# Delta-rule attention and two expert layers on one core: the first group's 32x32 inverse from two half blocks, and key products of groups 3 to 5 in the first two groups

## What is computed

```python
for t in range(S):                      # S = 768, for each batch (4) and head (8)
    y[t] = q[t] @ state
    v_old = k_n[t] @ state              # k_n is k over its norm
    state = state + beta[t] * outer(k_n[t], v[t] - v_old)
x = y                                    # [3072, 384]
P = sinkhorn(exp(x @ w_gate))            # 8 rounds
x = sum(P[:, e] * (relu(x @ w1[e]) @ w2[e]) for e in range(8))
h = x @ w_in
out = (h * cos(h)) @ w_out
```

## Time and profile before

| | us |
|---|---|
| median of 3 runs | 2217.05 (2216.68 to 2217.41) |
| the profiled execution | 2218.46 |
| its span, first to last instruction | 2216.7 |
| TensorE busy in the span | 2155.7 (97%) |
| VectorE busy | 1029.2 (46%) |
| ScalarE busy | 699.0 (32%) |

### The profile page before, as it was taken

How to read it: one execution, slowest core, us unless ns; L and a number is a source line. 1 busy time by engine, 2 the same in 40 slices (tenths; PEclk the granted TensorE clock), 3 DMA queues, 4 the chain that set the end, 5 groups by cost and what they waited for, 6 DMA issues and landing times.

```text
span 2216.7 us, 40360 instructions
## 1 busy us (share of the span) xinstructions
PE 2155.7 (97%) x15513; PEld 1778.8 (80%) x15513; DVE 1029.2 (46%) x1744; ACT 699.0 (32%) x1178; POOL 507.9 (23%) x404
## 2 busy tenths in 40 slices
PE   6789999999999999999999999999999999999999
PEld 5667778888888888888888888888888888888887
DVE  8988726432232322323223232232322348777777
ACT  4555543111111111111111111111111137666665
POOL 1000010045232332323323233232232330000000
PEclk7799999999999999999999999999999999999999
DMA  6334432011111011111111101111111100000001
GB/s 160 96 91 106 112 113 81 29 54 43 29 30 32 29 31 45 29 32 28 33 28 28 47 28 33 28 28 33 28 33 43 29 24 15 15 15 15 0 15 71
DMA packets 83113, 97.69 MB, mean 44 GB/s; under 512 B 6848, under 2 KB 68608, under 8 KB 83008
## 3 DMA queue, kind: packets, MB, share of 16 engines
q1 hardware_dynamic: 83008, 96.18, 15.8%
HBM read 82.69 MB, written 8.75 MB: 41 GB/s over the span
## 4 chain that ended last, share of the span: by engine, by line
PE 89%; DVE 9%; issue 1%; ACT 1%; DVEq 0%; ACTq 0%
PE h L712 7%; PE h L714 7%; PE h L713 7%; PE p_h L712 7%; PE p_h L714 7%; PE p_h L713 7%; PE am_y L751 4%; PE am_y L750 4%; PE am_y L752 4%; PE cy_y_y L750 4%; PE cy_y_y L751 4%; PE cy_y_y L752 4%; DVE t_leaf L1375 2%; DVE prod L1373 2%; PE o_y L750 2%; PE state_y L750 2%
## 5 line engine op out<-in xcount | busy, mean ns | idle before, releaser
L1278 POOL TENSOR_TENSOR acc<-acc,py 128x512 f32 (+1 forms) x252 | 324.3, 1318 | 745.8 <-DVE py L1585 745.8
L1143 ACT ACTIVATE hhi<-h 128x512 fp32r<-128x512 f32 x182 | 109.0, 599 | 770.8 <-PE h L714 770.8
L1548 DVE SCALAR_TENSOR_TENSOR hlo<-h,hhi 128x512 fp32r<-128x512 f32 x182 | 125.8, 691 | 474.6 <-ACT hhi L1143 474.6
L1548 DVE SCALAR_TENSOR_TENSOR hlo<-p_h,hhi 128x512 fp32r<-128x512 f32 x182 | 125.8, 691 | 403.6 <-ACT hhi L1143 403.6
L1240 POOL TENSOR_TENSOR wlo<-stage,whi (+1 forms) x114 | 147.0, 1291 | 628.8 <-ACT whi L1000 603.4
L712 PE MATMUL p_h<-xhi,whi 128*128 (+1 forms) x690 | 268.8, 390 | 0.6 <-DVE scr L1645 0.6
L712 PE MATMUL h<-xhi,whi 128*128 (+1 forms) x690 | 268.7, 389 | 0.0
L713 PE MATMUL p_h<-xlo,whi 128*128 (+1 forms) x690 | 268.5, 389 | 0.0
L714 PE MATMUL p_h<-xhi,wlo 128*128 (+1 forms) x690 | 268.4, 389 | 0.0
L713 PE MATMUL h<-xlo,whi 128*128 (+1 forms) x690 | 268.4, 389 | 0.0
L714 PE MATMUL h<-xhi,wlo 128*128 (+1 forms) x690 | 268.4, 389 | 0.0
(11 more groups left out here) (254 smaller groups left out, 3786.1 us busy)
## 6 DMA issues: line engine op xcount, KB each, us to landing
stage<-wcat SPq DMA_DIRECT2D x38, 768.0 KB, 4.4
pb<-p_scratch SPq DMA_DIRECT2D x84, 256.0 KB, 4.7
kq<-kqt SPq DMA_DIRECT2D x48, 192.0 KB, 3.5
v<-vrow SPq DMA_DIRECT2D x24, 192.0 KB, 3.9
kb<-krow SPq DMA_DIRECT2D x24, 192.0 KB, 3.6
acc<-yT SPq DMA_DIRECT2D x144, 32.0 KB, 2.1
kT<-kta SPq DMA_DIRECT2D x20, 192.0 KB, 4.5
acc<-y_scratch SPq DMA_DIRECT2D x5, 768.0 KB, 4.7
```

The source lines that it names most:

```text
L1143: act.activation(hhi[:, j, :], hps[j % 2][:, 0:TILE], ACT.Relu).then_inc(s["hhi_done"], 1)
L1278: pool.tensor_tensor(y, y, py[:, d, :], ALU.add).then_inc(s["added"], 1)
L1548: dve.scalar_tensor_tensor(out=hlo[:, j, :], in0=hps[j % 2][:, 0:TILE], scalar=0.0, in1=hhi[:, j, :].bitcast(F32), op0=ALU.max, op1=ALU.su ...
```

## The change

The first group's leaves are inverted in another way. Each 32x32 leaf is taken as two 16x16 diagonal blocks and the 16x16 block below them. VectorE inverts both diagonal blocks at once (half_blocks, a view with the two blocks as one more dimension), TensorE forms the lower block, in both layouts: joins multiplies the keys' product by the first half of z_t, ScalarE copies that into join scaled by a column of zeros and ones (lower), lower_blocks and turned_blocks multiply by z_x, and VectorE subtracts the results from z_t (lower_fixed) and z_x (turned_fixed). The three merges ahead of the first step are interleaved. GpSimd clears t_leaf and join first. The other five groups keep the 31-column elimination.

AHEAD is 3: TensorE computes key products of groups 0 to 2 in the lead. Those of 3 to 5 are placed by two tables, beside the residual of a step or after its outputs. ScalarE copies them out at the same places. In the lead, seven products of zeros (keep_up) stand where unread ones stood later; UNREAD keeps two entries, and unread waits for key copies and the first weights. The first three splits of weights and the gate's copy go from the lead to the end of step (0, 2) on ScalarE, the gate's subtraction to (1, 1) on VectorE. root(1) moves into step (0, 0), and the fourth quarter of extract(1) behind the third merged copy. The diff, cut:

```diff
-AHEAD = NG - 2
-NEAR_END = 2 + 1 + 2 * 26
-UNREAD = {(0, 0): (0, 3), (0, 1): (5, 0), (0, 2): (5, 0), (0, 3): (4, 0),
-          (1, 0): (4, 0), (1, 1): (5, 0), (1, 2): (5, 0)}
+HL = L // 2
+AHEAD = NG // 2
+KEYS_BESIDE = {(0, 1): (3, 1), (0, 2): (4, 1), (1, 0): (5, 0), (1, 1): (5, 1)}
+KEYS_AFTER = {(0, 0): (3, 0), (0, 1): (4, 0)}
+UNREAD = {(0, 3): 4, (1, 2): 5}
...
@@ sync
         for part in range(2):
-            load_kT(3, part)
+            load_kT(AHEAD, part)
         load_kq(2)
+        load_rows(2)
         load_w(0, 1, wraw)
-        load_rows(2)
         load_rows(3)
-        for part in range(2):
-            load_kT(AHEAD, part)
...
-                if g == 0 and c < 2:
-                    load_kT(NG - 1, c)
...
                 if c % 2 == 1:
                     move_y(i // 2)
+                if g == 0 and c < 2:
+                    for part in range(2):
+                        load_kT(AHEAD + 1 + c, part)
@@ tensor
+        def joins(bank, first, last):
+            for n in range(first, last):
+                for q in range(4):
+                    r, f = slice(L * q, L * q + L), L * (q % 2)
+                    mm = pe.matmul(bank[r, n * HL:(n + 1) * HL], keyed(0, n // RU)[r, n % RU, f:f + L], z_t[r, n, 0:HL],
+                                   start=True, stop=True)
+            mm.then_inc(a["join_made"], 1)
+
+        def lower_blocks(bank, first, last):
+            for n in range(first, last):
+                for q in (0, 2):
+                    r = slice(L * q, L * q + L)
+                    mm = pe.matmul(bank[r, n * HL:(n + 1) * HL], z_x[r, n, :], join[r, n, 0:HL], start=True, stop=True)
+            mm.then_inc(a["low_done"], 1)
+
+        def turned_blocks(bank, first, last):
+            for n in range(first, last):
+                for q in range(4):
+                    r = slice(L * q, L * q + L)
+                    mm = pe.matmul(bank[r, n * HL:(n + 1) * HL], join[r, n, :], z_x[r, n, HL:L], start=True, stop=True)
+            mm.then_inc(a["turned_done"], 1)
+
+        def first_inverses():
+            pe.wait_ge(a["zeroed"], 2)
+            pe.wait_ge(a["zt_half"], 1)
+            joins(cy_ps[:, 0, :], 0, 8)
+            joins(state_ps, 8, U)
+            pe.wait_ge(a["zx_first"], 1)
+            pe.wait_ge(a["join_evac"], 1)
+            pe.wait_ge(a["a_evac"], 4 * AHEAD)
+            lower_blocks(cy_ps[:, 1, :], 0, 8)
+            turned_blocks(o_ps, 0, 8)
+            pe.wait_ge(a["join_evac"], 2)
+            turned_blocks(am_ps[1], 8, 16)
+            pe.wait_ge(a["zt_fixed"], 1)
+            merge_units(0, 0, h_ps, 0, 8).then_inc(a["m_first"], 1)
+            lower_blocks(am_ps[0], 8, U)
+            pe.wait_ge(a["zx_fixed"], 1)
             pe.wait_ge(a["m_firsted"], 1)
-            merge_units(0, 1, h_ps, 0, 8).then_inc(a["m_first"], 1)
+            merge_units(0, 1, cy_ps[:, 0, :], 0, 8).then_inc(a["m_first"], 1)
+            turned_blocks(h_ps, 16, U)
+            pe.wait_ge(a["zt_fixed"], 2)
+            merge_units(0, 0, o_ps, 8, 16).then_inc(a["m_first"], 1)
...
         def unread(n):
+            pe.wait_ge(a["a_evac"], 4 * (NG - 1))
+            pe.wait_ge(s["whi_done"], 1)
             for _ in range(n):
                 pe.matmul(o_ps[:, :], w1(whi, 0, 0, 0), whi0[:, 0:TILE], start=True, stop=True)
+        def keep_up(n):
+            pe.wait_ge(a["zeroed"], 2)
+            zeros = X[:, 1, :, :].rearrange("p n i -> p (n i)")
+            for _ in range(n):
+                pe.matmul(cy_ps[:, 0, 0:2 * P], zeros[:, 0:P], zeros[:, P:3 * P], start=True, stop=True)
...
         query_products(0)
-        for g in range(2, AHEAD):
-            for m in range(2):
-                key_products(g, m)
-        pe.wait_ge(a["a_evac"], 4 * AHEAD)
-        pe.wait_ge(s["whi_done"], 1)
-        pe.wait_ge(a["leaf_chain"], NEAR_END)
-        unread(12)
-        first_merges()
-        unread(4)
+        pe.wait_ge(a["x_zeroed"], 1)
+        keep_up(4)
+        for m in range(2):
+            key_products(2, m)
+        keep_up(3)
+        first_inverses()
@@ scalar
         for r in range(4):
             products(1, r)
+        extract(1, 0, 3)
         for r in range(4):
             products(2, r)
-        extract(1)
-        for chunk in range(NT // 2):
-            split_hi(0, chunk, 0, 0, wraw)
-        for g in range(3, AHEAD):
-            for r in range(4):
-                products(g, r)
...
+        act.wait_ge(a["join_made"], 1)
+        joined(cy_ps[:, 0, :], 0, 8)
+        act.wait_ge(a["join_made"], 2)
+        joined(state_ps[:, :], 8, U)
         act.wait_ge(a["m_first"], 1)
...
+        act.wait_ge(a["m_first"], 3)
+        merged_units(0, 0, o_ps, 8, 16).then_inc(a["m_firsted"], 1)
+        extract(1, 3, 4)
...
+                if g == 0 and c == 2:
+                    act.wait_ge(s["gate_loaded"], 16)
+                    act.activation(wgr[:, :, 0, :], wgs[:, :, :], ACT.Copy).then_inc(s["gate_hi"], 1)
+                    for chunk in range(NT // 2):
+                        split_hi(0, chunk, 0, 0, wraw)
@@ vector
+        def half_blocks():
...
+            leaf_link(dve.tensor_tensor(t_half, a_half, turned(bpn.rearrange("p (a j) -> p a j", j=HL), HL), ALU.mult))
+            for j in range(1, HL - 1):
+                r = HL - 1 - j
+                t = t_half[:, :, j + 1:HL, 0:j]
+                x = prod[:, 0:2 * r * j].rearrange("p (a i c) -> p a i c", a=2, c=j)
+                leaf_link(dve.tensor_tensor(x, t_half[:, :, j + 1:HL, j:j + 1].broadcast_to([P, 2, r, j]),
+                                            turned(t_half[:, :, j, 0:j], r), ALU.mult))
+                leaf_link(dve.tensor_tensor(t, t, x, ALU.add))
...
+            dve.transpose(z_of[:, 0:HL, :], t_of[:, 0:HL, :]).then_inc(a["zt_half"], 1)
+            dve.transpose(z_x[:, :, :].rearrange("p n i -> p i n"), t_leaf[:, :, :]).then_inc(a["zx_first"], 1)
+            dve.transpose(z_of[:, HL:L, :], t_of[:, HL:L, :]).then_inc(a["zt_half"], 1)
...
         norms(0)
-        leaf_init(0)
-        leaf(1, 28)
-        leaf(28, L - 1)
-        leaf_end(0)
+        half_blocks()
+        lower_fixed(0, cy_ps[:, 1, :], 0, 8)
+        turned_fixed(0, o_ps[:, :], 0, 8)
         values(0)
+        lower_fixed(1, am_ps[0][:, :], 8, U)
+        turned_fixed(1, am_ps[1][:, :], 8, 16)
+        turned_fixed(2, h_ps[:, :], 16, U)
...
         leaf_start(1)
```

More of the change, by code:

```diff
@@ L158, in build @@
     r = [xlo_at]
-    t_leaf = inside(r, "t_leaf", [P, L, L])
+    t_leaf, t_half = leaf_buffer(r, "t_leaf")
     prod = inside(r, "prod", [P, 256])
@@ L173, in build @@
     assert r[0] <= xlo_at + 4 * EARLY * DC * TILE
+    lower = place("lower", [P, 2, L], F32, lgT_at)
+    join = place("join", [P, U, L], F32, xlo_at + 4 * DC * TILE + 4 * STEPS * HEADS * HD + 4 * HEADS * HB)
     mask_all = place("mask_all", [P, P], F32, xlo_at + 4 * DC * TILE + 4 * STEPS * HEADS * HD)
@@ L455, in key_products @@
                         k = kT[b * CT:b * CT + HD, (2 * m + c) * HEADS + par * HH + n, :]
-                        mm = pe.matmul(rows(key_bank(g, 2 * m + par), b ^ par)[:, j * CT:(j + 1) * CT], k, k, start=True, stop=True)
+                        mm = pe.matmul(rows(key_bank(2 * m + par), b ^ par)[:, j * CT:(j + 1) * CT], k, k, start=True, stop=True)
             mm.then_inc(a["a_done"], 2)
@@ L663, in step @@
                 merge(0, 3)
-            if AHEAD + g < NG and c < 2:
-                key_products(AHEAD + g, c)
+            if (g, c) in KEYS_AFTER:
+                key_products(*KEYS_AFTER[g, c])
             if c >= 2 and g + 1 < NG:
@@ L926, in scatter, with joined @@
                 scatter_units(g, q, part * 16, part * 16 + 16).then_inc(a["sc_done"], 1)
+        def joined(bank, first, last):
+            act.activation(join[:, first:last, 0:HL], bank.rearrange("p (n i) -> p n i", i=HL)[:, first:last, :], ACT.Copy,
+                           scale=lower[:, 1, 0:1]).then_inc(a["join_evac"], 1)
         def merged_units(g, stg, bank, first, last):
@@ L1090, in _ @@
                     scatter(0, 1)
[L1091 to L1093 removed]
+                if (g, c) in KEYS_AFTER:
+                    key_group, m = KEYS_AFTER[g, c]
+                    products(key_group, 2 * m)
+                    products(key_group, 2 * m + 1)
                 if c == 1 and g >= 1:
@@ L1228, in _ @@
                            pattern=[[-1, N_EXP]], channel_multiplier=1).then_inc(s["consts"], 1)
+        pool.memset(t_leaf[:, :, :], 0.0).then_inc(a["t_zeroed"], 1)
+        pool.memset(join[:, :, :], 0.0).then_inc(a["join_zeroed"], 1)
         pool.memset(X[:, :, :, :], 0.0).then_inc(a["x_zeroed"], 1)
@@ L1432, in _ @@
             dve.tensor_copy(mask[b * CT:(b + 1) * CT, :], mask_all[b * CT:(b + 1) * CT, b * CT:(b + 1) * CT]).then_inc(a["mask_cut"], 1)
+        dve.wait_ge(a["lower_made"], 2)
+        dve.transpose(lower[:, 1, :], lower[:, 0, :]).then_inc(a["lower_turned"], 1)
         first_extract(1)
```

127 lines of the change are left out of this document (79 added, 48 removed).

## The result

The changed kernel takes 2231.33 us (median of 4 runs, 2230.12 to 2232.15), the kernel before 2216.86 in the same series (2216.26 to 2217.41): 1.0065 times as long, 95% interval 1.0047 to 1.0082. It is slower by 14.5 us, where 2.4 us less were forecast. The profiled execution took 2232.15 us, its span 2230.4.

What follows compares the result with a forecast made beforehand. The scan of attention was taken as bound by VectorE, the rest by TensorE. A gain of 3.4 us at leaf_start(1) less 1.0 in (0,3) gave 2.4: 2217.05 to 2214.7 us, range 2209.5 to 2220.0.

Steps and rivals of the forecast that it cites:

- VectorE's list: First group's inverse on VectorE: elimination 7.8 us in place of 21.6; VectorE alone at leaf_start(1) 12.6 us early.
- half blocks don't do what they say on VectorE: Rival: each of the 28 elimination instructions pays 0.12 us more, 3.4 us, giving 2218.1 us; chance 0.06.
- the term of TensorE's stage: Joins to third merge on TensorE: records sum to 11.7 us, third merge at 38.4, gain 4.7 us before deductions.
- the deduction for its instruction stream: TensorE standing with nothing to wait for during the 736 records: 0.8 us, bounds 0 and 3.
- the bound that I named for the low clock: TensorE's small matmuls in the new stage: 26 ns a record at 1.2 GHz.
- TensorE becomes the bound and is slow: Rival: joins stage at 26 ns a record loses 2.8 us, 3 more in (0,3), 2222.9 us; chance 0.12.
- leaf_start(1) as the end of VectorE's wait: VectorE's leaf_start(1), waiting for ScalarE's extract, comes at 40.0 before deductions against 44.67; gain 3.4 us after them.
- the deductions: Taken off the stage's 4.7 us gain: 0.5 for low clock after TensorE's pause, 0.8 for its instruction stream.
- the moves: Key products, loads, splits and fill matmuls placed elsewhere: all at zero, except a 1.0 us loss in step (0,3).
- my upper bound of 3: Step (0,3), waiting for the first weight split: 3 us lost if the pauses stay and the clock falls.
- VectorE's saving should arrive at the end: Attention scan: every microsecond VectorE's list comes forward early reaches the end, unless a TensorE or ScalarE wait eats it.
- the forecast lead at R(0,1): Start of the residual in step (0,1): early by the same amount as leaf_start(1), 3.4 us.

Runs made afterwards that it cites:

- e1_root: Changed kernel with ScalarE's root(1) ahead of its wait for the second merge in step (0,0); 2228.67 us, 1.0050 of before.
- e3: Changed kernel with the first group's old 31-column inverse and root(1), extract(1) as before, all other moves kept; 2222.38 us, 1.0027 of before.
- e9: e3 with the gate's copy and first three weight splits back in the lead on ScalarE; 2219.81 us, 1.0014 of before.
- e15: e14 with the old 31-column inverse, so without the filled gap, its other places kept; 2217.11 us, 1.0002 of before.
- e14: e11 with key products spread over group 1, no last fill matmuls, both loads of keys 5 behind step (1,0); 2213.85 us, 0.9984 of before.
- e5: Changed kernel with VectorE doing group 1's work between its subtractions, later loads held back, splits in the lead, root(1) moved; 2220.52 us, 1.0011 of before.
- e8: e5 without lower_blocks, z_t taken from z_x by three VectorE transposes, 128 records fewer; 2216.57 us, 1.0000 of before.
- e10: Changed kernel with 64 more unread matmuls, 128 records, between joins and the first lower_blocks; 2234.29 us, 1.0078 of before.
- e2_loads: Changed kernel with five input loads issued only behind step (0,0); 2227.65 us, 1.0048 of before.
- e6: e5 without the filling, masked(0) ahead of lower_fixed(1), root(1) ahead of the second merge's wait; 2222.20 us, 1.0025 of before.
- e11: e8 with extract(2) moved behind updates(0, 2) on ScalarE; 2216.35 us, 0.9996 of before.
- e13: e11 with key products spread, no last fill matmuls, the load for (5,1) ahead of step (1,1)'s moves of y; 2219.37 us, 1.0006 of before.

## Why the prediction was wrong

**Right: VectorE's list.** The elimination was put at 7.8 us and took 7.8 (16.70 to 24.50), z_t's first half was to be ready at 26.5 and the joins to begin at 26.7 (26.6 and 26.73); subtractions of 128 and 256 elements were put at 0.3 and 0.45 and took 0.29 and 0.42. The rival "half blocks don't do what they say on VectorE" is out.

**Wrong: the term of TensorE's stage, and in it the deduction for its instruction stream.** The third merge was to end at 38.4; it ended at 50.2, 11.8 us later. Of that, 10.0 us are the four pauses, against a deduction of 0.8 with a bound of 3. The other 1.8 are the pace between them: 13.5 us for 736 records, 18.4 ns each, against 15.9. The four-quadrant records did what I took (91 in 1.41 us, 15.5 ns, even at a clock of 0.50); the two-quadrant ones, 83 in 2.19 us from 43.04, took 26 ns, the bound that I named for the low clock. I had the right row in hand, with pauses of 1.84 and 0.94 us, and took from it a sum for the whole stage, where it should have been read as a rate: between the ends of the two pauses, 89.87 and 93.84, before has 128 records as well. The windows of after between the ends of pauses show the rate (from:to, length, PE busy (count), PEclk, DMA share, GB/s):

```profile
26.70:34.67 7.97, 2.38 (x163) 0.50 0.96 270
34.67:38.56 3.89, 2.33 (x128) 0.50 0.03 11
38.56:42.02 3.46, 1.90 (x128) 0.50 0.02 5
42.02:48.93 6.91, 5.56 (x255) 0.50 0.02 5
```

128 records between one pause and the next, and 3.5 to 3.9 us for them; in the last row, two such blocks, the first with the slow two-quadrant records fills its 3.4 us itself and has only 0.08 us of pause behind it. So it is a rate, not a toll for each block. My own rival put the decision at 22 ns a record; the supply gives 27, and with the first pause the stage came to 32 (23.5 us for 736). So *TensorE becomes the bound and is slow* is what happened in place and sign, but in the main by a mechanism it did not have (supply; of its 26 ns at the low clock only the two-quadrant records took their part), and with 2222.9 us it was short by 8.4. It had 0.12.

**Wrong: leaf_start(1) as the end of VectorE's wait.** The stage handed on its 10.5 us (41.3 forecast with the deductions, 51.80 measured), but norms(1) lost another 4.1. root(1) moved into step (0,0), and there it stands on ScalarE behind the copy of the second merge; that merge stands on TensorE behind query_products(1), which writes the bank that masked(0) reads, and masked(0) stands behind leaf_start(1). I had listed the moved root(1) among the parts and costed none of what it was moved behind. e1_root won back 3.8 of the 4.1 at norms(1).

**Wrong in size: the moves.** Forecast: nothing, and 1.0 us in (0,3). R(0,3), R(1,0) and R(1,1) lose 1.0, 1.5 and 0.7 us in after; in run times e3 puts the moves at 5.3 us and e9 half of that, 2.6, at the splits in (0,3). The place was right: the fill matmuls ahead of TensorE's residual product there wait for the split, and the product behind them, in the timeline of after

```profile
97.06 1.65 ACT L1065 ACTIVATE whi<-wraw 128x512 fp32r<-128x512 f32 x3
...
97.81 1.62 PE L625 MATMUL o_y<-whi 128*128 128x512 f32 x3 [2.19 <-ACT whi L1065]
```

and the price is nearer to my upper bound of 3 than to the 1.0 that I took. That bound was for the case that the pauses stay and the clock falls, and both fit: a pause of 1.10 us stands in the S products right ahead of R(1,0) and one of 1.12 ends at 112.51, and the mean clock from 94.9 to 260 us is 0.91 instead of 0.97. What of the remaining 2.7 us is clock and what is copies beside the columns, no run separates. That the moves need not cost anything is shown by e15: with the splits in the lead, the key products spread further and keys 5 loaded in time, it is level with before.

**Right but worth nothing: "VectorE's saving should arrive at the end".** After the scan hardly anything is lost or won (R of the last step +14.3, time +14.5), and e14 hands its 4.5 us on (4.2 in the medians). But the 12.6 us by which VectorE alone is early arrive at best as 4: with the gap filled (e5, e8), R(0,1) is set by TensorE.

**In sum**: 10.5 (stage) + 4.1 (root) - 0.2 = 14.4 against the forecast lead at R(0,1), and 2.3 more than forecast in the steps to (1,2): 16.7 us, from -2.4 to +14.3.

## What to carry to other kernels

Before work is handed from an engine that is busy to one that is "half idle", count its instructions, not its busy time: here 128 records of small fp32 matmuls took 3.4 to 4.0 us a block, though TensorE was busy for only 1.9 to 2.3 us of it in most. Look for pauses with no releaser in the profile of before, count the records between them, and treat the result as a rate. A load moved out of the way of one stage can land on the next: e5's did. When an instruction is moved, write down what stands ahead of it in the new place on its engine and what that in turn waits for; and when a step is made earlier, look next at the loads whose issue is tied to the end of a step.

## What the runs showed of the hardware

**Instructions arrive in packets, and TensorE waits for them.** The DMA rows of after from 36 to 44 us (40 slices of 0.2 us: share in tenths, GB/s; then the packets by queue):

```profile
GB/s 0 82 0 0 0 0 0 0 0 0 0 0 0 0 0 0 0 0 82 0 0 0 0 0 0 0 0 0 0 0 0 0 0 0 0 82 0 0 0 0
DMA packets 3, 0.05 MB, mean 6 GB/s; under 512 B 0, under 2 KB 0, under 8 KB 0
...
q8 instruction: 3, 0.05, 2.3%
```

Nothing moves there but three packets of the instruction queue, at 36.3, 39.7 and 43.1 us, of 16 KB each (82 GB/s for 0.2 us); the next two are at 46.6 and 50.0. TensorE starts again at 38.57, 42.03, 45.48 and 48.94, each 2.3 to 2.4 us behind a packet, and the next packet comes 1.0 to 1.1 us after it has started. So with the DMA engines empty, 128 records still take a turn of some 3.45 us, 27 ns a record: the same 3.44 us that e10 paid for 128 records. The turn is not always that short: 3.89 us from 34.67 in after and 4.01 from 34.44 in e5, with a DMA share of 0.02 to 0.03. While the input loads run, a packet comes late. The rows of after from 28 to 36 us:

```profile
DMA  8999969999999999899999888999973211000000
...
q8 instruction: 1, 0.02, 0.8%
```

The engines are some 0.9 busy until 33.6, and the only packet of instructions between 25 and 36 us comes at about 32.2; TensorE starts again 2.5 us later, at 34.68. That is the pause of 5.57 us. With the loads moved, in e2_loads, the packet comes at 28.3 and the pause is 1.99. The last turn shows the same the other way round: 3.46 us in after with empty DMA engines, 5.11 in e5 and 5.39 in e6, where the loads that were held back run under it (shares 1.01 and 1.00). That the packet waits in line behind the loads' packets fits both, but its request is not in the trace.

The Trainium skill (Runtime: NRT & Kernel Launch, "Instruction fetch mechanics") says that an engine's instructions are refilled in blocks of 16 KiB, 256 instructions, by a DMA queue of its own, and that the cost of crossing a block is "mostly hidden". The trace agrees with the block: 128 matmul records with their 128 weight loads per packet. It does not agree with hidden: 1.3 to 1.6 us a block here, and 5.6 under load. The Trainium skill says also (TensorE: Matmul & The Clock Gate, "Wait — 56ns, not 53.3ns?") that matmuls start no closer than about 25 ns; in the bursts they start 31 ns apart (two records of 15.5), and over whole blocks 54 ns, so that rule did not bound anything here.

**The clock stays low in such a stage.** TensorE is at 1.00 from 20 to 24 us of after, under key products and keep_up, stands from 24.2 us to the joins at 26.73, and is at 0.50, 1.2 GHz, from 28 to 60; the bursts between the pauses don't bring it back: the mean clock from 24 to 60 us is 0.54, before it was 0.69. The four-quadrant records still came at the 15 ns that I had taken, the two-quadrant ones at 26 ns where I had taken 17.7.

**Still open**: what sets the 3.45 us of a turn, and whether it would be shorter at the high clock, since nearly all of the stage ran at the low one wherever the half blocks were in; and why e3, e5 to e8, e11, e13 and e14 spread over 6 to 12 us in ten or eleven runs, where before spread over 3 to 7 in 14 to 25.
